# Two heads in one 64x64 product at the 16- and 32-row levels of a block inverse, with every odd head's 16-row blocks reversed

## The reference

```python
for t in range(S):
    kt, vt, bt = (k_n[:, :, t], v[:, :, t], beta[:, :, t, None])
    y[:, :, t] = np.einsum('bhd,bhde->bhe', q[:, :, t], state)
    v_old = np.einsum('bhde,bhd->bhe', state, kt)
    state = state + bt[:, :, :, None] * np.einsum('bhd,bhe->bhde', kt, vt - v_old)
...
x = _moe_ref(x=x, **moe_kwargs)
return _moe2_ref(x=x, **moe2_kwargs)
```

## Time and profile before

| | us |
|---|---|
| median of 3 runs (1449.1 to 1450.45) | 1449.23 |
| the profiled execution | 1440.21 |
| its span (first to last instruction) | 1438.4 |
| before the loop and period 0, to 90 us | 90 |
| the loop's periods 1 to 11, to about 340 us | 250 |
| expert layers, from about 340 us | 1098 |

### The profile page before, as it was taken

How to read it: one execution, slowest core, us unless ns; L and a number is a source line. 1 busy time by engine, 2 the same in 40 slices (tenths; PEclk the granted TensorE clock), 3 DMA queues, 4 the chain that set the end, 5 groups by cost and what they waited for, 6 DMA issues and landing times.

```text
span 1438.4 us, 37111 instructions
## 1 busy us (share of the span) xinstructions
PE 1383.0 (96%) x14209; PEld 1269.0 (88%) x14210; DVE 1029.6 (72%) x1924; ACT 345.9 (24%) x811; POOL 376.3 (26%) x462
## 2 busy tenths in 40 slices
PE   5889999998999999998999999999999999999996
PEld 4789999987999999987899999999999999999996
DVE  5567777655566666668777777777777777777775
ACT  2345555442031001113111112111111111111111
POOL 1000101013253344466121212121222122222225
PEclk6999999999999999999999999999999999999999
DMA  5645554344433333100000000000000000000003
GB/s 116 138 95 113 121 108 117 80 132 148 151 111 111 111 105 111 35 28 12 12 23 11 22 11 22 11 22 11 22 11 22 11 22 11 22 11 22 11 16 116
DMA packets 101978, 85.70 MB, mean 60 GB/s; under 512 B 57520, under 2 KB 93488, under 8 KB 101872
## 3 DMA queue, kind: packets, MB, share of 16 engines
q1 hardware_dynamic: 84464, 51.52, 14.6%
q10 hardware_dynamic: 14336, 22.95, 5.0%
q0 software_dynamic: 3072, 9.71, 1.9%
HBM read 67.97 MB, written 16.18 MB: 59 GB/s over the span
## 4 chain that ended last, share of the span: by engine, by line
PE 86%; DMA 4%; DVE 3%; SPq 2%; issue 2%; ACT 2%; POOL 1%; ACTq 0%; POOLq 0%; DVEq 0%
PE bank L999 23%; PE bank L1001 23%; PE bank L1000 23%; PE bank L757 10%; PE bank L1035 2%; PE bank L885 2%; PE bank L888 1%; PE bank L905 1%; DMA inverse_blocks<-inverse 1%; ACT R L1195 1%; POOL out_dram L751 1%; DMA kq_sb<-in_kq_dram 1%; SPq L465 1%; PE bank L1006 1%; DVE sums L1835 1%
## 5 line engine op out<-in xcount | busy, mean ns | idle before, releaser
L1850 DVE SCALAR_TENSOR_TENSOR y_all<-bank,aux_all,y_all 128x384 f32<-128x384 f32 x360 | 217.9, 615 | 102.5 <-PE bank L1001 100.3
L1835 DVE TENSOR_TENSOR sums<-bank,sums 128x512 f32<-128x512 f32 x336 | 223.6, 688 | 58.8 <-PE bank L1001 45.7
L1395 ACT ACTIVATE gTh<-sums 128x512 fp32r<-128x512 f32 x192 | 110.9, 624 | 614.4 <-PE bank L1001 610.6
L999 PE MATMUL bank<-v2h,gTh 128*128 128x384 f32 x768 | 257.3, 335 | 1.4 <-DVE y_all L1850 0.7
L1001 PE MATMUL bank<-v2h,gTl 128*128 128x384 f32 x768 | 257.2, 335 | 0.0
L1000 PE MATMUL bank<-v2l,gTh 128*128 128x384 f32 x768 | 256.9, 334 | 0.0
L634 POOL TENSOR_TENSOR w_split_sb<-w_raw,w_split_sb 128x384 fp32r<-128x384 f32 (+1 forms) x98 | 110.4, 1188 | 155.4 <-ACT w_split_sb L1349 142.9
L999 PEld LDWEIGHTS bank<-v2h,gTh 128*128 128x128 f32 x768 | 144.2, 188 | 3.9 <-DVE y_all L1850 1.0
L1000 PEld LDWEIGHTS bank<-v2l,gTh 128*128 128x128 f32 x768 | 144.2, 188 | 1.8
L1001 PEld LDWEIGHTS bank<-v2h,gTl 128*128 128x128 f32 x768 | 144.1, 188 | 0.0
L1839 DVE SCALAR_TENSOR_TENSOR gTl<-sums,gTh 128x512 fp32r<-128x512 f32 x192 | 139.4, 767 | 4.9 <-ACT gTh L1395 1.6
(11 more groups left out here) (239 smaller groups left out, 2788.6 us busy)
## 6 DMA issues: line engine op xcount, KB each, us to landing
w_raw<-in_moe_w_dram ACTq DMA_DIRECT2D x13, 1536.0 KB, 7.1
xs_in<-x_rows SPq DMA_DIRECT2D x31, 203.0 KB, 2.4
v_raw<-in_moe_w_dram SPq DMA_DIRECT2D x15, 384.0 KB, 3.2
kq_sb<-in_kq_dram SPq DMA_DIRECT2D x28, 192.0 KB, 3.7
kt_sb<-in_kt_dram SPq DMA_DIRECT2D x24, 196.0 KB, 3.3
vt_sb<-in_vt_dram SPq DMA_DIRECT2D x24, 192.0 KB, 4.3
vA_raw<-in_moe_w_dram SPq DMA_DIRECT2D x15, 256.0 KB, 2.6
kq_sb<-in_kq_dram SPq DMA_DIRECT2D x14, 256.0 KB, 5.0
```

The source lines that it names most:

```text
L999: pe.matmul(dst, lh, rh, start=first, stop=False)
L1395: act.activation(sum_place(gTh, k), sums[:, SUM_TILE[k]], ACT.Relu).then_inc(g_hi, 1)
L1835: dve.tensor_tensor(out_, x, y, ALU.add).then_inc(sum_ok, 1)
L1850: dve.scalar_tensor_tensor(out=a, in0=src, scalar=share, in1=a, op0=ALU.mult, op1=ALU.add).then_inc(acc_ok, 1)
```

## The change

It puts two neighbouring heads, 2g and 2g+1, into one 64x64 product of a level. On the host every odd head's 16-token blocks are reversed in each chunk (k, v and beta; q is not), so that at a level the blocks of the odd head that are solved and known lie in the places that the even head leaves free. Each of the four level products has 16 products instead of 32 (8 values of g, `NG`, and two halves `a`). For that the left factor must hold columns of both heads: ACT builds it from R in new steps `level16_rows` (four activations of 128 partitions x 8 x 16) and `level32_rows` (two of 128 x 8 x 32), with a column of zeros and ones (`marks16`, `marks32`) as the scale. They write two new tiles, `R16` and `R32`. In the loop they stand for chunk c+2 behind `left32_taken(c+1)`; before it, for chunk 0 ahead of `left16_taken(0)`, and for chunk 1 behind `gram_scaled(2, 1)`. The wait of `gram_scaled` on `z32_mm` goes. `X16` and `Z32` shrink or stay at 128 x 512; `blocks_turned` has two transposes of 128 x 256 in place of one of 128 x 1024; `level16_taken` has two plain additions of 128 x 256 in place of two scaled ones, and needs no mask column. `query_masked` takes a mask of 128 columns, with the rows of the odd head in reversed blocks. The two memsets of `Z16` and `Z32` on POOL and ACT's wait for them go.

```diff
             def level16_left(n):
-                pe.wait_ge(r_ok, 2 * n + 2)
+                pe.wait_ge(r16_ok, n + 1)
                 pe.wait_ge(x16_ok, n + 1)
                 if n >= 1:
                     pe.wait_ge(y32_ok, n)
-                for h in range(NPAIR):
+                for g in range(NG):
                     for a in HALVES:
-                        last = mul(level_out(a, h), R[half_rows(a), n % NR, h], two_heads(X16, a, h, 0, BS))
+                        last = mul(level_out(a, g), R16[half_rows(a), g], X16[half_rows(a), g])
                 last.then_inc(z16_mm, 1)
 
             def level16_right(n):
                 pe.wait_ge(z16_ok, n + 1)
-                for h in range(NPAIR):
+                for g in range(NG):
                     for a in HALVES:
-                        last = mul(level_out(a, h), Z16[half_rows(a), h], two_heads(Y[:, n % NY], a, h, BS, 2 * BS))
+                        last = mul(level_out(a, g), Z16[half_rows(a), g], solved16(Y[half_rows(a), n % NY], g))
                 last.then_inc(y16_mm, 1)
 
             def level32_left(n):
+                pe.wait_ge(r32_ok, n + 1)
                 pe.wait_ge(x32_ok, n + 1)
-                for h in range(NPAIR):
+                for g in range(NG):
                     for a in HALVES:
-                        last = mul(level_out(a, h), R[half_rows(a), n % NR, h], X32[half_rows(a), with_next(h)])
+                        last = mul(level_out(a, g), R32[half_rows(a), g], X32[half_rows(a), g])
                 last.then_inc(z32_mm, 1)
...
             def gram_scaled(n, p):
                 act.wait_ge(gain_ok, n + 1)
-                if n >= NR:
-                    act.wait_ge(z32_mm, n - NR + 1)
...
+            def level16_rows(n):
+                act.wait_ge(r_ok, 2 * n + 2)
+                if n >= 1:
+                    act.wait_ge(z16_mm, n)
+                for v in range(4):
+                    cols, known = slice(BS * v, BS * v + BS), v ^ 1
+                    last = act.activation(R16[:, :, cols], R[:, n % NR, (v + 1) % 2::2, cols], ACT.Copy, scale=marks16[:, known:known + 1])
+                last.then_inc(r16_ok, 1)
+
+            def level32_rows(n):
+                if n >= 1:
+                    act.wait_ge(z32_mm, n)
+                for b in range(2):
+                    cols = slice(2 * BS * b, 2 * BS * b + 2 * BS)
+                    last = act.activation(R32[:, :, cols], R[:, n % NR, (b + 1) % 2::2, cols], ACT.Copy, scale=marks32[:, 1 - b:2 - b])
+                last.then_inc(r32_ok, 1)
...
             squares(3)
-            act.wait_ge(eye_ok, 2)
+            act.wait_ge(const_in, 16)
+            level16_rows(0)
+            level32_rows(0)
             left16_taken(0)
...
                 if onward:
                     left32_taken(c + 1)
+                if c + 2 < NC:
+                    level16_rows(c + 2)
+                    level32_rows(c + 2)
                 if c >= 1:
                     logits_taken(c - 1)
...
             def blocks_turned(n):
...
-                dve.transpose(X16[:], Y[:, n % NY]).then_inc(x16_ok, 1)
+                for b in range(2):
+                    ins = dve.transpose(X16[:, :, 2 * BS * b:2 * BS * b + 2 * BS], known16_of(Y[:, n % NY], b))
+                ins.then_inc(x16_ok, 1)
 
             def level16_taken(n):
                 dve.wait_ge(y16_mm, n + 1)
-                src = bank[2][:].rearrange("p (h b x) -> p h b x", b=2, x=BS)
-                for b, sign in ((0, first_rows), (1, third_rows)):
-                    at_ = Y[:, n % NY, :, 32 * b + BS:32 * b + 2 * BS]
-                    ins = dve.scalar_tensor_tensor(out=at_, in0=src[:, :, b, :], scalar=sign, in1=at_, op0=ALU.mult, op1=ALU.add)
+                src = bank[2][:].rearrange("p (g b q x) -> p g b q x", b=2, q=2, x=BS)
+                for b in range(2):
+                    at_ = solved16_of(Y[:, n % NY], b)
+                    ins = dve.tensor_tensor(at_, at_, src[:, :, b], ALU.add)
                 ins.then_inc(y16_ok, 1)
```

More of the change, by code:

```diff
@@ L82, in fused_kernel @@
         strict_up = const_sb[:, 128:256]
-        strict_half = const_sb[:, 256:320]
-        first_rows = const_sb[:, 320:321]
-        third_rows = const_sb[:, 321:322]
+        strict_half = const_sb[:, 256:384]
+        marks16 = const_sb[:, 384:388]
+        marks32 = const_sb[:, 388:390]
         ones = place("ones", [128, 128])
@@ L112, in fused_kernel @@
         kt_sb = place("kt_sb", [128, NKT, KW])
-        X16 = place("X16", [128, NPAIR, CH])
+        X16 = place("X16", [128, NG, CH])
+        cursor[0] += 4 * NG * CH
         length = place("length", [128, NC, NPAIR])
@@ L119, in fused_kernel @@
         Y = place("Y", [128, NY, NPAIR, CH])
-        Z16 = place("Z16", [128, NPAIR, CH])
-        Z32 = place("Z32", [128, NPAIR, CH])
+        Z16 = place("Z16", [128, NG, CH])
+        Z32 = place("Z32", [128, NG, CH])
+        R16 = place("R16", [128, NG, CH])
+        R32 = place("R32", [128, NG, CH])
         err = place("err", [128, NPAIR, D])
@@ L222, in fused_kernel, with in_twos, solved16, solved16_of @@
         bank = [ctx.enter_context(nc.psum_tensor(f"bank{i}", [128, 512], f32)) for i in range(8)]
+        def in_twos(x):
+            return x.rearrange("p (g o) i -> p g (o i)", o=2)
+        def solved16(x, g):
+            return bass.AP(x.tensor, x.offset + 2 * CH * g + BS, [x.ap[0], [2 * BS, 2], [3 * BS, 2], [1, BS]])
+        def solved16_of(x, b):
+            return bass.AP(x.tensor, x.offset + 2 * BS * b + BS, [x.ap[0], [2 * CH, NG], [3 * BS, 2], [1, BS]])
+        def known16_of(x, b):
+            return bass.AP(x.tensor, x.offset + 2 * BS * b, [x.ap[0], [2 * CH, NG], [5 * BS, 2], [1, BS]])
+        def solved32(x):
+            return in_twos(x)[:, :, 2 * BS:6 * BS]
+        def known32(x):
+            return bass.AP(x.tensor, x.offset, [x.ap[0], [2 * CH, NG], [6 * BS, 2], [1, 2 * BS]])
         cleared = sem("cleared")
@@ L251, in fused_kernel @@
         y0_in = [sem(f"y0_in{i}") for i in range(NY)]
+        r16_ok = sem("r16_ok")
+        r32_ok = sem("r32_ok")
         x16_ok = sem("x16_ok")
@@ L834, in level32_right @@
                 pe.wait_ge(z32_ok, n + 1)
-                for h in range(NPAIR):
+                for g in range(NG):
                     for a in HALVES:
-                        last = mul(level_out(a, h), Z32[half_rows(a), h], Y[half_rows(a), n % NY, with_next(h), 32:64])
+                        last = mul(level_out(a, g), Z32[half_rows(a), g], solved32(Y[half_rows(a), n % NY])[:, g])
                 last.then_inc(y32_mm, 1)
@@ L1279, in _ @@
             gram_scaled(2, 1)
+            level16_rows(1)
+            level32_rows(1)
             def inverse_cleared(c):
@@ L1961, with odd_reversed @@
     n_c, n_p = S // C, B // 2
+    def odd_reversed(x):
+        x = x.copy()
+        x[:, 1::2] = x[:, 1::2].reshape(B, H // 2, n_c, C // 16, 16, -1)[:, :, :, ::-1].reshape(x[:, 1::2].shape)
+        return x
+    k, v, beta = odd_reversed(k), odd_reversed(v), odd_reversed(beta)
     def by_dim(x):
@@ L1971 @@
     upper = (ramp[:, None] < ramp[None, :]).astype(_np.float32)
-    half = _np.concatenate([upper[:C, :C], upper[:C, :C]])
-    first = (ramp % C < 16).astype(_np.float32)[:, None]
-    third = ((ramp % C >= 32) & (ramp % C < 48)).astype(_np.float32)[:, None]
+    half = _np.concatenate([upper[:C, :C], upper[:C, :C].reshape(C // 16, 16, C)[::-1].reshape(C, C)], axis=1)
+    half = _np.concatenate([half, half])
+    marks = [(ramp[:, None] % C // n == _np.arange(C // n)).astype(_np.float32) for n in (16, 32)]
     gates = _np.concatenate([inputs['moe_w_gate'], inputs['moe_w_output_gate']], axis=1)
@@ L1980 @@
         'beta': beta.reshape(n_p, 2, H, n_c, C).transpose(1, 4, 3, 0, 2).reshape(2 * C, n_c * n_p * H),
-        'const': _np.concatenate([_np.eye(128, dtype=_np.float32), upper, half, first, third], axis=1),
+        'const': _np.concatenate([_np.eye(128, dtype=_np.float32), upper, half] + marks, axis=1),
         'gates': gates.reshape(-1, 128, gates.shape[1]).transpose(1, 0, 2),
```

30 lines of the change are left out of this document (12 added, 18 removed).

## The result

The changed kernel takes 1424.68 us (median of 4 runs, 1420.42 to 1426.23), the kernel before 1449.2 (4 runs). The direction was right, and so were the two limits behind TensorE; the size was not.

What follows compares the result with a forecast made beforehand. PE was taken to bind the attention loop, with SP's queue and the q loop close behind. 8.4 + 2.8 + 0.4 + 2.0 - 1.5 = 12.1 us off 1440.21 gives 1428.1, plus 9 carried over: 1437.1, range 1426 to 1445.

Steps and rivals of the forecast that it cites:

- the two limits behind TensorE: Attention loop: SP's own work with its landings, 22.6 us a period, and the q-DVE-SP loop of waits, 23.73 us.
- 9 us above it for a reason that no row shows, and I carry the difference over: Last step: the runs' median, 1449.23, against the profiled 1440.21; the difference was added to 1428.1, giving 1437.1.
- The period: Attention loop: 23.2 us, the middle of both limits, against 24.40; 1.2 us saved seven times, 8.4 us.
- the rival in which PE stays the bound: Nothing else ends last; chunks 2 to 11 each give 3.70: 37 us, 1412. Chance 0.10.
- `level16_right` ends before DVE comes to need it: Loop of waits through q: no level product that gets shorter lies in its 23.73 us.
- Before the loop: Chunk 0's `level16_left` waits for four activations, copy 0.6 us late, `level16_right` gives 0.9 back: taken as zero, bounds 1 us.
- Tail: From period 8 on: 2.8 us from shorter level products, 0.4 from the transpose, 2.0 in period 10; 5.2 in all.
- The clock's charge: Granted clock falls to 0.50 after PE's waits, mostly inside PE's slack; charged once, 1.5 us lost.
- the 22.6 that I had counted for SP alone: Attention loop: SP's own work with its landings, 24.40 - 1.8 = 22.6 us a period, unchanged by the change.
- ACT: Six added activations ahead of `gram_scaled`: 2.1 us, bounds 0.58 and 11.5, just fitting the 2.3 us left.
- DVE: Two transposes of 256 for one of 1024: 0.36 us less together; plain sums cost no more than 0.479 each.
- The rule of LDWEIGHTS busy share: Attention loop: PEld busy 22.37 of 24.15 us, 93%; by the rule PE binds and the change pays in full.

Runs made afterwards that it cites:

- g0_before: The kernel before, unchanged, run and profiled once more in the third group of runs: 1449.38 us.
- e0_before: The kernel before, unchanged, profiled once more in the first group of runs: 1441.61 us, ratio 1.000.

## Why the prediction was wrong, point by point

*What failed* is the step "9 us above it for a reason that no row shows, and I carry the difference over". Up to there the sum gave 1428.1 for the changed kernel, and it takes 1424.7, 1427.5 and 1429.2. The 9 us are no constant on top of both kernels. Most of them are stops of TensorE in one group of 64 records: this group takes 3.67 us instead of 1.95 in five of seven periods, while PE is what a period waits for. With 32 records it takes 1.04 us in the same surroundings. What both kernels do carry over is the 2.0 us in the expert layers. My own trace held the warning: the profiled execution was 9 us under all three timed runs, which agreed within 1.4 us. Such a gap belongs to some stage, and if that stage is the one that is changed, it isn't carried over. As a term it was worth 7 x (25.41 - 24.32) = 7.6 us in the seven periods. Compared at one level, the run g0_before against the profile after, the sum closes: 101.05 - 99.58 = 1.5 us before chunk 3's mark, 177.85 - 160.78 = 17.1 in the seven periods, 77.9 - 71.7 = 6.2 from there to the first cast, and 0.1 in the expert layers: 24.8, and 24.5 were measured. The forecast had 0 for the 1.5, 8.4 for the 17.1, and 5.2 less 1.5 for the 6.2.

*The period*: forecast 23.2 us, measured 22.97 and 23.34 from mark to mark. The two limits behind PE, SP's queue and the loop through q, were right, and so was the rejection of the rival in which PE stays the bound: the seven periods gave 9.4 us against the profile of before (forecast 8.4), not 26. One step of the loop was right only for the level of that profile: "`level16_right` ends before DVE comes to need it". At the high level DVE waits 1.1 to 1.4 us for this product in five of the seven periods of g0_before.

*Before the loop*: forecast 0, measured 102.81 - 99.58 = 3.2 us profile to profile. But e0_before, the same file at the same level as the profile of before, has this mark at 100.44, 2.4 us earlier, and at the high level the difference is 1.5 to 2.4. So the term is above 0 and not well known; together with the 4 us of the run with chunks 0 to 2 halved, my bound of 1 us was too tight. That the four shorter products of the first chunks count, in a prologue in which ACT's copies delay only one of them, is argued.

*Tail*: forecast 5.2, less 1.5 for the clock. From chunk 10's mark to the first cast it took 350.3 - 273.0 = 77.3 us before and 332.1 - 260.4 = 71.7 after: 5.5 before rounding. The clock's charge falls in the seven periods: the one shown above is 25.00 - 22.63 = 2.4 us over the mean of the others, and 4 to 5 us in the two other profiles of the changed kernel. So charging it once was right and 1.5 us too little; the late landing of q ahead of it has a part in these figures that can't be split off. Without that period the mean is 22.63 us, the 22.6 that I had counted for SP alone. The mean granted clock of the span fell from 0.986 to 0.978. The 2.0 us in the layers behind, in which I had expected no change, are the two levels of the profiles; at one level the difference is 0.1 and 0.8 us. The sum profile to profile is 3.2 + 9.4 + 5.5 - 2.0 = 16.1.

*ACT*: six activations 1.98 us against 2.1, slack 0.29 against 0.2; the run with them twice shows that the slack really ends there. *DVE*: two transposes and two sums, nothing that can be measured. *The rule of LDWEIGHTS busy share* (the Trainium skill, Perfetto Trace Analysis, Identifying the Most-Contended Engine) named the engine whose relief pays: all of the gain is TensorE's. How much it pays it didn't say: PE's busy time shrank by 31.9 us and the span by 16.2.

What stays open: what makes TensorE stop there in some groups of runs and not in others, why at this group, and what the changed kernel takes at the low level.

## What to carry to other kernels

When the profiled execution lies outside the timed runs, find the stage that differs before adding the gap to a forecast; if the change relieves that stage, the gap is part of the gain. When an engine binds by a hair (1.5 us of 24 here), work out the limits behind it, since they set the new period to some tenths of a us whatever is taken from the first. And time a kernel in more than one group of runs: the same file stood at 1441 and at 1450 us, each time within 6 us of the median. A stage that the change doesn't touch tells whether two profiles may be set side by side: here the expert layers, 1088.1 us at one level and 1090 at the other.

## What the runs showed of the hardware that I had not expected

TensorE can stop with nothing shown that it waits for, at nearly the same instruction of an unrolled loop in period after period, for 0.4 us two or three times, after some 48 records at full pace. The pages of the two profiled kernels also show what the change takes from the supply of instructions (queue: loads, MB, share):

```profile
q8 instruction: 79, 1.29, 0.4%
```
```profile
q8 instruction: 67, 1.10, 0.3%
```

These are 12 loads of 16 KB less, as many as there are chunks. Both kernels before, with and without the stops, have the same 79. The Trainium skill, Runtime: NRT & Kernel Launch, Instruction fetch mechanics, says that the sequencer streams instructions in 16 KiB blocks and that crossing a boundary is mostly hidden. The sizes agree (1.29 MB / 79 = 16 KB); whether the stops are such crossings no run here shows. The loads at least don't keep step with them: in the five groups with stops in g0_before a load starts 0.2, 2.0, 2.9, 2.0 and 2.4 us behind the group's start, while the last stop ends 3.3 us behind it in every one.

Second, TensorE's signals can come later than its records end, and here they do so at one level only. The same file, the kernel before with half of all level products, at the low level (e1_half) and at the high one (i3_half): `level16_right` of the last chunk, and DVE's `level16_taken`, which has long been waiting for it.

```profile
297.08 1.14 PE L757 MATMUL bank<-Y,Z 64*64 64x64 f32 x32
298.26 0.87 DVE L1519 SCALAR_TENSOR_TENSOR Y<-bank,const_sb,Y 128x256 f32<-128x256 f32 x2 [4.73 <-PE bank L757]
```
```profile
292.29 1.14 PE L757 MATMUL bank<-Y,Z 64*64 64x64 f32 x32
295.67 0.88 DVE L1519 SCALAR_TENSOR_TENSOR Y<-bank,const_sb,Y 128x256 f32<-128x256 f32 x2 [6.93 <-remote]
```

DVE goes on 1.2 us behind the group's start at the low level and 3.4 us behind it at the high one. The changed kernel's profile, in the loop, has the same:

```profile
115.08 1.11 PE L786 MATMUL bank<-Y,Z 64*64 64x64 f32 x32
...
118.37 0.34 PE L908 MATMUL bank<-state,kq_sb 64*64 64x64 f32 x4 [0.16 <-issue]
...
118.53 0.75 DVE L1566 TENSOR_TENSOR Y<-Y,bank 128x256 f32<-128x256 f32 x2 [0.99 <-remote]
```

Its 32 records had ended by 116.2, and DVE goes on at 118.53, 3.45 us behind the group's start. Wherever DVE waits for a halved `level16_right` at the high level, in eight profiles, it is 3.4 to 3.5 us; with 64 records and stops it is 3.8 to 4.0. The row at 118.37 is PE's own share: it has a gap that ends 3.3 us behind the group's start, just where the last stop of the 64-record group ends, only that by now PE is in `read_out`. So halving the group doesn't take the late moment away. It takes most of its price away: from the group's start to the last record of that `read_out` it costs PE 4.6 us instead of 4.2, where the kernel before takes 6.9 instead of 5.1. The ends of matmuls in the trace are modelled, so what PE does between 116.2 and 118.4 isn't known; the start of DVE's instruction isn't modelled.
